# A mixture of experts whose two matrix products per tile are interleaved with those of the tile in front

## The reference, cut to what matters

```python
def _moe_ref(x, w_gate, w_output_gate, w1, w2):      # x (3072, 384), w1 (8, 384, 1024), w2 (8, 1024, 384)
    e_idx = np.argmax(x @ w_gate, axis=1)
    ...
    for e in range(E):
        mask = e_idx == e
        h = np.maximum(x[mask] @ w1[e], 0.0)
        ye = h @ w2[e]
        out[mask] = gate_w[mask, None] * eom[mask, e, None] * ye
```

## Time and profile before

| what | us |
|---|---|
| median of 3 runs | 1198.79 |
| lowest and highest of them | 1197.86, 1202.87 |
| the profiled execution, its own time | 1203.62 |
| its span in the profile | 1201.9 |
| TensorE busy | 1030.9 (86%) |
| VectorE, ScalarE, GpSimd busy | 480.0, 365.8, 327.6 |
| granted TensorE clock, mean | 0.955 |

### The profile page before, as it was taken

How to read it: one execution, slowest core, us unless ns; L and a number is a source line. 1 busy time by engine, 2 the same in 40 slices (tenths; PEclk the granted TensorE clock), 3 DMA queues, 4 the chain that set the end, 5 groups by cost and what they waited for, 6 DMA issues and landing times. The chain is left out here.

```text
span 1201.9 us, 31001 instructions
## 1 busy us (share of the span) xinstructions
PE 1030.9 (86%) x13236; PEld 895.3 (74%) x13237; DVE 480.0 (40%) x922; ACT 365.8 (30%) x732; POOL 327.6 (27%) x226
## 2 busy tenths in 40 slices
PE   1699999999999999603988998899959999999999
PEld 1588788888887787502877887788848887888888
DVE  3355555555555554332234323433334233242322
ACT  0245445555545455200212212212222122121211
POOL 2222333232333220084255045531630001000000
PEclk9979999999999999755999999999979999999999
DMA  8712122122111110043333244412320101100000
GB/s 267 270 29 60 29 56 55 43 60 60 29 56 38 40 34 3 1 156 127 138 116 113 85 144 137 144 42 103 111 66 20 45 28 33 33 20 27 7 20 27
DMA packets 59389, 86.29 MB, mean 72 GB/s; under 512 B 29200, under 2 KB 54288, under 8 KB 56720
## 3 DMA queue, kind: packets, MB, share of 16 engines
q1 hardware_dynamic: 53616, 48.46, 12.7%
q0 software_dynamic: 5664, 36.18, 8.9%
HBM read 61.82 MB, written 22.81 MB: 70 GB/s over the span
## 5 line engine op out<-in xcount | busy, mean ns | idle before, releaser
L1009 PE MATMUL hb<-early,last_h 128*128 128x512 f32 x648 | 203.8, 396 | 4.7 <-ACT o_sb L1123 3.6
L1009 PEld LDWEIGHTS hb<-early,last_h 128*128 128x128 f32 x648 | 120.5, 189 | 30.8 <-ACT o_sb L1123 2.7
L1009 PE MATMUL hb<-early,last_l 128*128 128x512 f32 x324 | 126.9, 392 | 0.0
L480 DVE TENSOR_TENSOR p<-bank,cf 128x512 f16<-128x512 f32 x96 | 66.0, 688 | 46.3 <-PE bank L283 46.0
L283 PEld LDWEIGHTS bank<-t,n_hi 64*64 64x64 f16 x2688 | 66.7, 111 | 22.8 <-issue 7.4
L931 POOL TENSOR_TENSOR late<-w_raw,late 128x3072 fp32r<-128x3072 f32 x8 | 59.7, 7459 | 73.6 <-DVE late L918 73.6
L1147 DVE TENSOR_TENSOR m<-hb,m 128x512 f32<-128x512 f32 x36 | 24.9, 692 | 131.4 <-PE hb L1009 131.4
L283 PE MATMUL bank<-t,n_hi 64*64 64x64 f16 x2688 | 72.0, 195 | 5.1 <-issue 4.3
L1009 PE MATMUL ob<-wo_h,early 128*128 128x384 f32 x288 | 74.2, 335 | 0.0
L881 ACT ACTIVATE h_sb<-h_bank 128x512 f32<-128x512 f32 x28 | 16.8, 598 | 186.5 <-PE h_bank L792 186.5
L792 PE MATMUL y_acc<-early,ht_h 128*128 128x384 f32 x240 | 63.4, 345 | 11.3 <-DVE ht_l L903 11.3
(11 more groups left out here) (157 smaller groups left out, 2258.8 us busy)
## 6 DMA issues: line engine op xcount, KB each, us to landing
w_raw<-w POOLq DMA_DIRECT2D x14, 1536.0 KB, 6.9
kq_t<-qh SPq DMA_DIRECT2D x24, 256.0 KB, 3.3
x_sorted<-zeros SPq DMA_DIRECT2D x32, 192.0 KB, 1.9
x_in<-x_sorted SPq DMA_DIRECT2D x29, 192.0 KB, 2.3
y_sorted<-y_sb SPq DMA_DIRECT2D x28, 192.0 KB, 1.9
k_raw<-kt_in SPq DMA_DIRECT2D x24, 192.0 KB, 3.3
k_own<-kh SPq DMA_DIRECT2D x24, 192.0 KB, 3.3
v_in<-vh SPq DMA_DIRECT2D x24, 192.0 KB, 3.5
```

What stands on the lines that cost most here:

```text
L480: dve.tensor_tensor(p16[st][:], pb, mask_of(lv), ALU.mult).then_inc(prod_out[st], 1)
L1009: ins = pe.matmul(out, a[x], b[y], start=first and i == 0, stop=last and i == 2, skip_group_check=True)
```

## The change

The tiles of `experts` become a pipeline on TensorE. For tile `g` it now does the first layer of `g`, the three transposes of the rows of `g + 1`, the first half of the second layer of tile `g - 1`, the eight transposes of `g`, and the second half of the second layer of `g - 1`. The second layer of the last tile stands alone behind the loops. The two halves of `ht` are still one buffer, so ScalarE waits for `y_done` of the tile in front before it writes the second half (`n == 1`). VectorE copies `y_acc` of tile `g - 1` between its two splits of `ht` of tile `g`.

The eight experts are written out on each engine. The first tile of each expert is written out too, and a loop runs over the rest, so there are sixteen copies of the tile's body. Only the end of an expert is loaded from `table`. The cast of raw `w1` stays at the start of the expert's first tile, that of raw `w2` moves to that tile's end. SyncE's stores are one tile later in its order. GpSimd's program is as before.

```diff
@@ of_experts
+        begin = 0
+        for e in range(E):
+            end = eng.value_load(table[0:1, 1, e:e + 1], min_val=1, max_val=MAXB)
+            tile(e, e % 2, begin, True)
+            with eng.Fori(begin + 1, end) as g:
+                tile(e, e % 2, g, False)
+            begin = end
+        return end
@@ SyncE
-        with sp.Fori(0, total - 1) as g:
+        for g in range(2):
+            sp.wait_ge(xt_done, g + 1)
+            sp.dma_start(x_in[:], xs[P * (g + 1):P * (g + 2), :]).then_inc(x_got, 16)
+        with sp.Fori(1, total - 1) as g:
             sp.wait_ge(xt_done, g + 2)
             sp.dma_start(x_in[:], xs[bass.ds(P * g + 2 * P, P), :]).then_inc(x_got, 16)
             sp.wait_ge(y_out, g + 1)
-            sp.dma_start(ys[bass.ds(P * g, P), :], y_sb[:]).then_inc(y_sent, 16)
...
+            sp.dma_start(ys[bass.ds(P * g - P, P), :], y_sb[:]).then_inc(y_sent, 16)
+        for i in range(2):
+            sp.wait_ge(y_out, total + i)
+            sp.dma_start(ys[bass.ds(P * total + P * (i - 2), P), :], y_sb[:]).then_inc(y_sent, 16)
@@ TensorE (hidden, transpose_h and output hold the lines of the old body)
+        def tile(e, par, g, first):
+            if first:
+                pe.wait_ge(weights.lo_ready[0], e + 1)
+            hidden(par, g)
+            transpose_x(g + 1)
+            if first and e == 0:
+                transpose_h(g)
+                pe.wait_ge(weights.lo_ready[1], 1)
+                return
+            of = 1 - par if first else par
+            pe.wait_ge(ht_lo[1], g)
+            output(of, 0)
+            transpose_h(g)
+            output(of, 1).then_inc(y_done, 1)
+            if first:
+                pe.wait_ge(weights.lo_ready[1], e + 1)
 
         transpose_x(0)
-        of_experts(pe, body, before)
+        total = of_experts(pe, tile)
+        pe.wait_ge(ht_lo[1], total)
+        output((E - 1) % 2, 0)
+        output((E - 1) % 2, 1).then_inc(y_done, 1)
@@ ScalarE
             for n in range(2):
                 act.wait_ge(ht_done[n], g + 1)
+                if n == 1 and not (first and e == 0):
+                    act.wait_ge(y_done, g)
@@ VectorE
+        def tile(e, par, g, first):
+            if first:
+                high_part(e, par, 0)
             dve.wait_ge(h_done[1], g + 1)
             dve.tensor_scalar(h_sb[:, 512:1024], h_bank[1][:, :], 0.0, None, ALU.max).then_inc(h_out[1], 1)
             split_x(g + 1)
...
+            split_h(g, 0)
+            if not (first and e == 0):
+                output(g)
+            split_h(g, 1)
+            if first:
+                high_part(e, par, 1)
```

More of the change, by code:

```diff
@@ L793, in three, with of_experts @@
         return ins
[L795 to L809, removed]
+    def of_experts(eng, tile):
+        begin = 0
[6 more added lines that the diff above has]
+        return end
     passed_pe, passed_pool, passed_sp = sem("passed_pe_x"), sem("passed_pool_x"), sem("passed_sp_x")
@@ L819, in _ @@
         total = sp.value_load(table[0:1, 1, E - 1:E], min_val=E, max_val=MAXB)
-        sp.wait_ge(xt_done, 1)
-        sp.dma_start(x_in[:], xs[P:2 * P, :]).then_inc(x_got, 16)
-        with sp.Fori(0, total - 1) as g:
+        for g in range(2):
+            sp.wait_ge(xt_done, g + 1)
+            sp.dma_start(x_in[:], xs[P * (g + 1):P * (g + 2), :]).then_inc(x_got, 16)
+        with sp.Fori(1, total - 1) as g:
             sp.wait_ge(xt_done, g + 2)
@@ L825, in _ @@
             sp.wait_ge(y_out, g + 1)
-            sp.dma_start(ys[bass.ds(P * g, P), :], y_sb[:]).then_inc(y_sent, 16)
-        sp.wait_ge(y_out, total)
-        sp.dma_start(ys[bass.ds(P * total - P, P), :], y_sb[:]).then_inc(y_sent, 16)
-        sp.wait_ge(y_sent, 16 * total + 1)
+            sp.dma_start(ys[bass.ds(P * g - P, P), :], y_sb[:]).then_inc(y_sent, 16)
+        for i in range(2):
+            sp.wait_ge(y_out, total + i)
+            sp.dma_start(ys[bass.ds(P * total + P * (i - 2), P), :], y_sb[:]).then_inc(y_sent, 16)
+        sp.wait_ge(y_sent, 16 * total + 17)
         sp.sem_inc(passed_sp, 1)
@@ L839, in transpose_x, with hidden @@
             ins.then_inc(xt_done, 1)
[L841 to L846, removed]
+        def hidden(par, g):
             pe.wait_ge(xt_hi, g + 1)
@@ L853, in body, with transpose_h @@
                 ins.then_inc(h_done[n], 1)
-            transpose_x(g + 1)
+        def transpose_h(g):
             for n in range(2):
@@ L860, in body, with output @@
                 ins.then_inc(ht_done[n], 1)
[L862 to L868, removed]
+        def output(par, n):
+            for c in range(4 * n, 4 * n + 4):
+                ins = three(pe, y_acc[:, 0:X], [t[:, c, :] for t in ht], [w[:, c, :] for w in w2s[par]],
+                            c == 0, c == KF - 1)
+            return ins
+        def tile(e, par, g, first):
[14 more added lines that the diff above has]
+                pe.wait_ge(weights.lo_ready[1], e + 1)
         transpose_x(0)
-        of_experts(pe, body, before)
+        total = of_experts(pe, tile)
+        pe.wait_ge(ht_lo[1], total)
+        output((E - 1) % 2, 0)
+        output((E - 1) % 2, 1).then_inc(y_done, 1)
     @block.scalar
@@ L877, in split_x @@
             act.copy(xt[0][:].rearrange("p c t -> p (c t)"), xt_bank[:, 0:X]).then_inc(xt_hi, 1)
-        def body(e, par, g):
+        def tile(e, par, g, first):
             act.wait_ge(h_done[0], g + 1)
@@ L884, in body @@
                 act.wait_ge(ht_done[n], g + 1)
+                if n == 1 and not (first and e == 0):
+                    act.wait_ge(y_done, g)
                 act.copy(ht[0][:, 4 * n:4 * n + 4].rearrange("p c t -> p (c t)"), ht_bank[n][:, :]).then_inc(ht_hi[n], 1)
         split_x(0)
-        of_experts(act, body)
+        of_experts(act, tile)
     @block.vector
@@ L895, in split_x, with split_h, output, high_part @@
                               xt[0][:].rearrange("p c t -> p (c t)"), ALU.subtract).then_inc(xt_lo, 1)
-        def body(e, par, g):
+        def split_h(g, n):
+            dve.wait_ge(ht_hi[n], g + 1)
+            dve.tensor_tensor(ht[1][:, 4 * n:4 * n + 4].rearrange("p c t -> p (c t)"), ht_bank[n][:, :],
+                              ht[0][:, 4 * n:4 * n + 4].rearrange("p c t -> p (c t)"), ALU.subtract).then_inc(ht_lo[n], 1)
+        def output(following):
+            dve.wait_ge(y_done, following)
+            dve.wait_ge(y_sent, 16 * following + 1)
+            dve.tensor_copy(y_sb[:], y_acc[:, 0:X]).then_inc(y_out, 1)
+        def high_part(e, par, i):
+            dve.wait_ge(weights.raw_again[i], 16 * e + 16)
+            if e == E - 1:
+                dve.tensor_copy(weights.last[i][0], weights.flat_raw(i)[:, 0:KX * F2]).then_inc(weights.last_hi[i], 1)
+            else:
+                dve.tensor_copy(splits[1 - par][i][0], weights.flat_raw(i)).then_inc(weights.hi_ready[i], 1)
+        def tile(e, par, g, first):
+            if first:
+                high_part(e, par, 0)
             dve.wait_ge(h_done[1], g + 1)
@@ L900, in body @@
             split_x(g + 1)
[L901 to L920, removed]
+            split_h(g, 0)
[4 more added lines that the diff above has]
+                high_part(e, par, 1)
+        dve.memset(y_sb[:, 0:1], 0.0).then_inc(y_sent, 17)
+        dve.memset(y_sb[:, 1:2], 0.0).then_inc(y_out, 1)
         split_x(0)
-        of_experts(dve, body, before)
+        total = of_experts(dve, tile)
+        output(total)
     @block.gpsimd
```

## The result

| what | before | after |
|---|---|---|
| median of the runs, us | 1200.83 (4 runs) | 1157.74 (4 runs) |
| lowest and highest | 1197.86, 1202.97 | 1153.47, 1167.4 |
| the profiled execution, its own time | 1203.62 | 1154.56 |
| its span | 1201.9 | 1152.8 |
| TensorE busy | 1030.9 (86%) | 1012.1 (88%) |

The ratio of after to before is 0.9654, 95% interval 0.9583 to 0.9725: the kernel is faster by 43 us. The forecast was 1157.6 us, in a range from 1152 to 1168. It was counted off the median of three runs before, 1198.79; a fourth run makes it 1200.83.

What follows compares the result with a forecast made beforehand. TensorE was taken to bound the kernel, with waits in the expert stage; 568.6 + 27 x 9.50 + 1.75 + 4.25 = 831.1 against 872.25 gave 41.2 us less, 1198.8 - 41.2 = 1157.6, range 1152 to 1168.

Steps and rivals of the forecast that it cites:

- The steady tile: Expert tiles on TensorE: 4.12 + 0.33 + 0.88 + 4.17 = 9.50 us, 1.29 less than 10.79; bounds 9.40 and 9.70.
- Both waits: TensorE's waits in each tile for VectorE's relu (0.26 us) and the low part of `ht` (0.82 us), to go.
- Both slacks: In a steady tile, relu 1.5 us early; second half of `ht` ready at 1.6 us, wanted at 4.45: 2.8 us.
- The first tile: Start of expert stage: TensorE waits for the next rows' low part, so tile 1's first layer starts at 568.6.
- The last tile: End of expert stage: second layer without cover, 1.75 us idle, then 4.25 us of matmuls.
- The expert starts: First tiles of experts: all 7.3 us extra go, the cast of `w1` ending just when the relu may start.
- The second rival: First tiles of experts: cast makes the relu 0.3 to 1.5 us late, 7 x 1.5 = 10; up to 1170; chance 0.07.
- The unrolled program: Written-out expert code: zero cost on TensorE; bound above 0.52 us at sixteen bodies, 8.3 us.
- New code stalling TensorE (1166): Sixteen written-out tile bodies: waits go, but each body stalls TensorE 0.52 us, 8.3 us in all; chance 0.08.
- The held relu (1170): First tiles of experts: VectorE's issue work and cast delay the relu beyond its slack; up to 1170; chance 0.07.
- The late `ht` (1192): Each tile: second half of `ht` 4.5 us late, TensorE waits as now, only expert starts gain 7 us; chance 0.03.
- The slower one, a fetch at each back edge: Each tile's loop branch on TensorE waits for code; at 2 us a tile 15 us slower, 1214; chance 0.02.

Runs made afterwards that it cites:

- e6: Changed kernel with ScalarE's copy of the second half of `ht` done seven times; expert stage 304.28 us against 272.09 in the changed kernel.
- e1: Kernel before with experts and first tiles written out, old order in a tile, both casts at the expert's start; 1192.83 us against 1202.93, ratio 0.9912.
- e7: Kernel before with its eight experts written out, one tile loop each, both bounds loaded; expert stage 308.50 us against 312.96 before.
- e8: Kernel before with its eight experts written out, one tile loop each, only each expert's end loaded; expert stage 305.64 us against 312.96 before.
- e3: Changed kernel with both casts at the end of the expert's first tile; expert stage 271.64 us against 272.09 in the changed kernel.
- e9: Changed kernel with two more register loads of each expert's end on each engine; expert stage 272.08 us against 272.09 in the changed kernel.
- e10: Changed kernel with six more register loads of each expert's end on each engine; expert stage 291.70 us against 272.09 in the changed kernel.
- e4: Changed kernel with the cast of `w1` done three times at each expert's start; expert stage 276.43 us against 272.09 in the changed kernel.

## Why the prediction was right, step by step

**The steady tile: right.** 9.50 us were forecast, 9.51 measured. Both waits are gone. The parts differ, in both directions: eight transposes take 0.79 and not 0.88, the row transposes 0.25 and not 0.33, and the two halves of the second layer take 2.18 + 2.16 and not 4.17. That the sum comes out within 0.01 us is luck: the short transposes make up for the longer second layer. Both slacks were read rightly off: `ht` is ready 1.6 us into the next tile and used at 4.4, and e6 shows that it is this slack (2.7 us). That TensorE's waits are the gain, and not the writing out, is shown by e1: 7.6 us without the new order, 33.3 more with it.

**The first tile: right.** The first layer of tile 1 was forecast 9.02 us behind the first `xt_l` (568.6 - 559.58). It starts 8.97 behind it in the changed kernel, right behind the low part that ends at 560.15:

```profile
559.59 0.56 DVE L905 TENSOR_TENSOR xt_l<-xt_bank,xt_h 128x384 fp32r<-128x384 f32 x1
...
560.29 0.70 PE L792 MATMUL h_bank<-early,xt_h 128*128 128x512 f32 x2
```

**The last tile: right.** 1.75 + 4.25 = 6.0 was forecast, and its y copy comes 5.89 behind the one in front, with 1.5 us of wait.

**The expert starts: right in size, the cause only in part.** The step "there VectorE does two casts (3.43 us) ahead of its relu, after 1.2 to 1.8 us in which it only issues" names both, and the change was to win by taking one cast away. e1 keeps both casts there and loses the 7.3 us all the same: with 0.3 us of issue gap, the casts and the relu just fit behind an idle VectorE. The shorter gap is thus enough by itself, and it comes from the loading of two bounds and the closing of the outer loop (e7, e8). Whether taking one cast away would have been enough with a gap of 1.2 us was not run. I had the gap in the earlier trace rows and carried it over into the new kernel unchanged; at the second expert's start it is 0.16 there, and the cast begins 1.7 us into the tile and not 2.6 to 2.8. That mistake cost nothing in the sum, because in the pipeline either would be hidden (e3, e9). For the same reason the gains do not add up: the pipeline would give the 7.3 us without the writing out as well. This is argued from e3 and e9; a pipeline in the old loops was not run.

The second rival also says that the first tiles other than the one from 639.44 have 0.7 us extra each. Four of them have 0.6 to 0.75, the last expert's has none, and the one at the other place where the outer loop jumps back has 1.37:

```profile
718.68 0.56 DVE L907 COPY y_sb<-y_acc 128x384 f32<-128x384 f32 x1 [4.00 <-PE y_acc L792]
721.05 3.43 DVE L918 CAST late<-w_raw 128x3072 fp32r<-128x3072 f32 x2 [1.81 <-issue]
...
730.84 0.56 DVE L907 COPY y_sb<-y_acc 128x384 f32<-128x384 f32 x1 [3.71 <-PE y_acc L792]
```

The issue gap is the same there as at 641.83 (1.81 and 1.83). The 1.6 us between the two tiles (12.16 and 13.76) go with the fall of the clock at the first of them; in the second it stayed at 1.00.

**The unrolled program: right.** No stall at new code: e1 and the changed kernel show none. The rule of the Trainium skill (page "Runtime: NRT & Kernel Launch", section "Instruction fetch mechanics") that a taken branch out of what is held waits for a fetch would fit the 0.95 us that the outer loop's close costs against e7, but these runs do not separate a fetch from the register work there.

**The rivals.** New code stalling TensorE (1166): did not come. e10 shows that TensorE can stand for want of instructions, but behind loads, and only beyond some 1.3 us more of them at a place; no run shows a stall by new code. The held relu (1170): did not come; e4 shows where it would begin. The late `ht` (1192): e6 is that case, and it shows an error in the rival's numbers. A half that is ready 4.5 us into the next tile is wanted at 4.45 and would cost next to nothing; e6, where it is ready 5.3 us into the tile, costs 1.0 us a tile, so the full 1.3 us of the old waits would need some 0.3 us more. The slower one, a fetch at each back edge: 27 tiles at 9.51 exclude it.

**The median.** 41.2 us were forecast off 1198.8. The stage gave 40.9. That the median fell on the forecast within 0.2 us is luck: the runs of the changed kernel spread over 14 us, and the measured difference of 43.1 us is 1.9 more than forecast because the median before rose by 2.0 with the fourth run.

## What to carry to other kernels

Read a steady tile's stretches from start to start, and price the same matmuls where another stage runs them without a gap: the difference is what a reordering can give; here the parts came out within 0.2 us each, and their sum closer by luck. Then write down for each wait when its data is ready and when the new order wants it; where the slack is 2 us, details such as the exact place of the transposes, or where a cast stands, do not matter, and need not be tuned. A gap marked as issue ahead of an instruction was here the loading of loop bounds and the closing of a loop; if other engines wait behind such a gap, it is worth removing before the instruction behind it is blamed.

## What was not expected of the hardware

One register load of a loop bound costs 0.6 us of issue time on VectorE (e7 against e8), as much as a pass over a 128x384 tile.

GpSimd's low part of a weight took 6.78 us or 8.14 us before and 6.80 always in the changed kernel. The rows of the changed kernel, instructions on `w_raw`, ns min/median/max:

```profile
L955 POOL DMA_DIRECT2D w_raw<-w x12: 551/1044/1714, 561.8 to 733.0; - x12
...
L951 POOL TENSOR_TENSOR late<-w_raw,late x8: 6763/6806/6825, 554.2 to 763.6; 128x3072 fp32r<-128x3072 f32 x8
L951 POOL TENSOR_TENSOR early<-w_raw,early x6: 6796/6804/6807, 592.6 to 725.5; 128x3072 fp32r<-128x3072 f32 x6
```

Before, the first low part began beside VectorE's second cast. Now no cast runs beside a low part; in exchange GpSimd's issue of the transfer falls beside the cast of `w2` and takes up to 1.71 us, where in the written-out kernel without the casts apart (e1) it took at most 0.58. The Trainium skill, page "SBUF — State Buffer", section "Who interferes with whom", describes VectorE and GpSimd as sharing one port pair, which a VectorE cast in a mode that uses both of its ports takes for the whole instruction, so that the other engine waits. The trace agrees, with 1.3 us more beside a cast that overlaps by about 1.5. It goes the other way as well: in e4, where the first low part is still running when VectorE casts `w2`, that cast takes 3.88 us and not 1.75, and ends 1.6 us behind the low part (609.45):

```profile
602.63 6.82 POOL L959 TENSOR_TENSOR early<-w_raw,early 128x3072 fp32r<-128x3072 f32 x1 [21.30 <-DVE early L931]
...
607.18 3.88 DVE L931 CAST early<-w_raw 128x3072 fp32r<-128x3072 f32 x1
```

None of this is on the path here: in e4 too the tiles in which it happens take 9.5 us.
